# Low-weight pass of the up projections on 64-row halves of the array, in a fused convolution and two MLPs

## The reference, cut to what matters

```
x = attn(x, weight).reshape(8192, 192)
h = x @ w_in1;  g = maximum(0.01 * h, h);  x = g @ w_out1
h = x @ w_in2
P = a[0] + a[1] * h + a[2] * h**2 + a[3] * h**3
Q = 1 + |b[0]| * |h| + |b[1]| * h**2
out = (P / (Q + 1e-6)) @ w_out2
```

## Time and profile before

| | us |
|---|---|
| median of 3 runs | 1404.3 |
| the profiled execution's own time | 1407.92 |
| its span on the core | 1406.1 |
| mean granted TensorE clock | 0.973 |
| PE busy | 1293.8 (92%) |
| PEld busy | 1035.3 (74%) |
| DVE busy | 1068.8 (76%) |
| ACT busy | 1048.8 (75%) |
| POOL busy | 627.8 (45%) |

### The profile page before, as it was taken

How to read it: one execution, slowest core, us unless ns; L and a number is a source line. 1 busy time by engine, 2 the same in 40 slices (tenths; PEclk the granted TensorE clock), 3 DMA queues, 4 the chain that set the end, 5 groups by cost and what they waited for, 6 DMA issues and landing times.

```text
span 1406.1 us, 14543 instructions
## 1 busy us (share of the span) xinstructions
PE 1293.8 (92%) x5724; PEld 1035.3 (74%) x5724; DVE 1068.8 (76%) x913; ACT 1048.8 (75%) x1075; POOL 627.8 (45%) x265
## 2 busy tenths in 40 slices
PE   6989999999999999999999999999999999999575
PEld 5768787777777777777777877777787777778453
DVE  3447877878687787868778786877878687787774
ACT  4557787777787787778778777887877777787563
POOL 0014544545445454544545444454544445454553
PEclk8899999999999999999999999999999999999886
DMA  8200000000000000000000000000000000000000
GB/s 202 55 1 12 0 12 13 1 24 1 24 1 12 13 0 24 0 25 0 12 13 1 24 0 24 0 12 13 0 24 0 24 1 12 0 1 12 0 12 11
DMA packets 25091, 21.73 MB, mean 15 GB/s; under 512 B 2909, under 2 KB 23997, under 8 KB 25023
## 3 DMA queue, kind: packets, MB, share of 16 engines
q1 hardware_dynamic: 25023, 20.80, 5.3%
HBM read 14.49 MB, written 6.30 MB: 15 GB/s over the span
## 4 chain that ended last, share of the span: by engine, by line
issue 47%; POOL 44%; PE 4%; ACT 2%; DMA 1%; DVE 1%; POOLq 0%; SPq 0%; ACTq 0%; DVEq 0%
POOL den L297 23%; POOL lo L303 21%; PE h L580 2%; DMA den<-in_moe_w_in 1%; DMA band<-tap_rows 0%; DVE lo L527 0%; ACT hi L385 0%; PE acc L599 0%; PE h L546 0%; PE acc L600 0%; PE acc L590 0%; PE acc L591 0%; PE acc L592 0%; DMA coef_b<-in_moe_b 0%; ACT h L381 0%
## 5 line engine op out<-in xcount | busy, mean ns | idle before, releaser
L580 PE MATMUL h<-xs,wa 128*128 128x512 f32 x2520 | 620.5, 397 | 66.6 <-DVE xs L474 27.9
L297 POOL TENSOR_TENSOR den<-den,rec 128x1024 f32<-128x1024 f32 x128 | 323.7, 2529 | 762.8 <-ACT den L372 762.8
L580 PEld LDWEIGHTS h<-xs,wa 128*128 128x128 f32 x2520 | 474.5, 191 | 191.6 <-DVE xs L474 34.7
L303 POOL TENSOR_TENSOR lo<-pol,rec 128x1024 fp32r<-128x1024 f32 x128 | 307.1, 2399 | 4.0 <-DVE pol L507 4.0
L489 DVE SCALAR_TENSOR_TENSOR hi<-pol,coef_a,rec 128x1024 fp32r<-128x1024 f32 x128 | 164.3, 1284 | 143.2 <-ACT rec L338 88.6
L527 DVE TENSOR_TENSOR lo<-h,hi 128x1024 fp32r<-128x1024 f32 x128 | 156.4, 1222 | 132.2 <-ACT hi L385 131.8
L599 PE MATMUL acc<-lo,wb 128*128 128x512 f32 x512 | 202.3, 395 | 18.3 <-POOL lo L303 18.3
L590 PE MATMUL acc<-hi,wb 128*128 128x512 f32 x512 | 208.8, 408 | 10.9 <-DVE out_cm L502 8.8
L381 ACT ACTIVATE h<-h 128x1024 f32<-128x1024 f32 x128 | 129.7, 1014 | 116.1 <-PE h L580 116.0
L357 ACT ACTIVATE rec<-h 128x1024 f32<-128x1024 f32 x124 | 127.3, 1027 | 108.0 <-PE h L580 107.3
L591 PE MATMUL acc<-hi,wb 128*128 128x512 f32 x512 | 202.3, 395 | 0.0
(11 more groups left out here) (76 smaller groups left out, 954.7 us busy)
## 6 DMA issues: line engine op xcount, KB each, us to landing
out<-out_tok SPq DMA_DIRECT2D x16, 384.0 KB, 2.6
x_tok<-in_x SPq DMA_DIRECT2D x64, 82.5 KB
pol<-in_moe_w_out SPq DMA_DIRECT2D x4, 384.0 KB, 10.8
x_tok<-in_x SPq DMA_DIRECT2D x16, 78.0 KB
den<-in_moe_w_in SPq DMA_DIRECT2D x2, 512.0 KB, 8.4
den<-in_moe_w_in SPq DMA_DIRECT2D x4, 256.0 KB, 8.5
rec<-in_moe_w_out SPq DMA_DIRECT2D x2, 384.0 KB, 10.4
den<-in_moe_w_out SPq DMA_DIRECT2D x2, 384.0 KB, 6.1
```

The source lines that it names most:

```text
L297: nc.gpsimd.tensor_tensor(den[k][:, :], den[k][:, :], rec[k][:, :], ALU.mult).then_inc(s_den, 1)
L303: nc.gpsimd.tensor_tensor(lo2[k][:, :], pol[k][:, :], rec[k][:, :], ALU.mult).then_inc(s_lo2, 1)
L580: last = T.matmul(dst[:, half, :], lhs, xs[m][:, part, :], start=(j == 0), stop=(j == 4))
```

## The change

Of each up projection the fifth matmul of both tiles is taken out of `up`. In its place, once a pair, come two matmuls over 64 rows each: the low weights of tile 0 from partitions 0 to 63 by a new copy of x high on partitions 0 to 63 (`rest_hi`), and the low weights of tile 1 from partitions 64 to 127 by x high where it already is. They write different PSUM banks. The product of low weights and low x, which the fifth matmul also gave, is no longer computed. The remaining four matmuls of a tile are `up_whole`, the pair of half-array matmuls is `up_rest`. In layer 2 `up_rest` comes last and in layer 1 first (except in phase 6, where it comes last there too), so that in ordinary steps the four half-array matmuls of both layers follow one another. ScalarE gets one more copy of 64 by 512 per block and layer; in phase 6 VectorE's second subtraction, and with it TensorE, waits for it. `tap_half`, a small row used before the first block, now shares the memory of `conv_sb`.

```diff
-        tap_half = sb("tap_half", [1, HEADS * ROW])
+        rest_hi = [sb(f"x_rest{m}", [DR, COLS], F32R)[:, :] for m in range(2)]
+        conv_row = conv_sb[:, :, :].rearrange("p a c -> p (a c)")
@@ ScalarE
                 nc.scalar.activation(xs[1][DR:P, 2, :], fold[DR:P, :], ACT.Copy).then_inc(s_x2_hi, 1)
+                nc.scalar.activation(rest_hi[1], fold[DR:P, :], ACT.Copy).then_inc(s_x2_rest, 1)
...
                 nc.scalar.activation(xs[0][DR:P, 2, :], xt_ps[DR:P, 1, ::-1], ACT.Copy).then_inc(s_xt_hi, 1)
+                nc.scalar.activation(rest_hi[0], xt_ps[DR:P, 1, ::-1], ACT.Copy).then_inc(s_xt_rest, 1)
@@ VectorE
-                dve.wait_ge(s_xt_hi, 2 * c + 2)
+                dve.wait_ge(s_xt_rest, c + 1)
@@ TensorE
-            def up(m, pair0, dst, rest_ready, done):
+            def up_whole(m, pair0, dst, opens, rest_ready, done):
...
-                    w = [wa[m][:, j, f * P:(f + 1) * P] for j in range(4)]
-                    terms = [(w[0], 0), (w[1], 0), (w[0], 1), (w[2], 2), (w[3], 2)]
+                    w = [wa[m][:, j, f * P:(f + 1) * P] for j in range(3)]
+                    terms = [(w[0], 0), (w[1], 0), (w[0], 1), (w[2], 2)]
...
+            def up_rest(m, pair0, dst, opens, done):
+
+                f = 2 * (pair0 % STEPS)
+                T.matmul(dst[:, 0, :], wa[m][0:DR, 3, f * P:(f + 1) * P], rest_hi[m], start=opens, stop=not opens)
+                last = T.matmul(dst[:, 1, :], wa[m][DR:P, 3, (f + 1) * P:(f + 2) * P], xs[m][DR:P, 2, :],
+                                start=opens, stop=not opens)
+                if done is not None:
+                    last.then_inc(done, 1)
...
-                    up(1, n, hidden_2(n), x2_rest_ready, s_h2)
+                    up_whole(1, n, hidden_2(n), True, x2_rest_ready, None)
+                    if phase == 0:
+                        pe.wait_ge(s_x2_rest, n // STEPS + 1)
+                    up_rest(1, n, hidden_2(n), False, s_h2)
...
                             if transposes:
+                                pe.wait_ge(s_xt_rest, m0 // STEPS + 1)
                                 pe.wait_ge(s_xt_lo, 2 * (m0 // STEPS) + 2)
-                        up(0, m0, hidden_1(n), xt_rest_ready, s_h1)
+                        if transposes:
+                            up_whole(0, m0, hidden_1(n), True, xt_rest_ready, None)
+                            pe.wait_ge(s_xt_hi, 2 * (m0 // STEPS) + 2)
+                            up_rest(0, m0, hidden_1(n), False, s_h1)
+                        else:
+                            up_rest(0, m0, hidden_1(n), True, None)
+                            up_whole(0, m0, hidden_1(n), False, xt_rest_ready, s_h1)
```

More of the change, by code:

```diff
@@ L103, in conv_mlp_mlp @@
         one = sb("one", [P, 1])
-        tap_half = sb("tap_half", [1, HEADS * ROW])
+        rest_hi = [sb(f"x_rest{m}", [DR, COLS], F32R)[:, :] for m in range(2)]
+        conv_row = conv_sb[:, :, :].rearrange("p a c -> p (a c)")
         out_row = out_cm[:, :, :].rearrange("p a c -> p (a c)")
-        tap_rows = [t[0:1, 0:HEADS * ROW].rearrange("p (h j) -> p h j", h=HEADS) for t in (tap_half, out_row)]
+        tap_rows = [t[0:1, 0:HEADS * ROW].rearrange("p (h j) -> p h j", h=HEADS) for t in (conv_row, out_row)]
         tap_dram = nc.dram_tensor("tap_rows", (H, ROW), F32, kind="Internal").ap()
@@ L156, in conv_mlp_mlp @@
         s_x2_lo = sem("x2_lo")
+        s_x2_rest = sem("x2_rest_doubled")
+        s_xt_rest = sem("xt_rest_doubled")
         s_abs = sem("abs_h")
@@ L579, in up @@
                             rest_ready()
-                        last = T.matmul(dst[:, half, :], lhs, xs[m][:, part, :], start=(j == 0), stop=(j == 4))
-                last.then_inc(done, 1)
+                        last = T.matmul(dst[:, half, :], lhs, xs[m][:, part, :], start=opens and j == 0,
+                                        stop=not opens and j == 3)
+                if done is not None:
[5 more added lines that the diff above has]
+                                start=opens, stop=not opens)
+                if done is not None:
+                    last.then_inc(done, 1)
             def down(m, pair0, hi, lo, lo_ready, done):
```

## The result

The changed kernel took 1419.28 us (median of 6 runs, 1415.65 to 1423.09) against 1403.86 us before. The ratio is 1.0113, 95% interval 1.0089 to 1.0136: slower, by 15.4 us. The profiled execution of the changed kernel has a span of 1420.9 us, 14.8 more than before.

A forecast was written before the change was run, and what follows sets the result against it. TensorE's matmul stream was taken to set the time nearly everywhere; 132 charges of 0.55 us less 43.6 us saved gave +29 us, 1437 for the profiled execution and a median of 1433 us, range 1396 to 1464.

The forecast's parts named there:

- Entering and leaving, 0.44 us: TensorE: switching from whole-array to half-array matmuls and back costs 0.22 us each way, 0.44 for both.
- The second half trails by 0.11 us: Half-array pair on TensorE: the second half's weight load follows the first's, so it trails by 0.11 us.
- 8 w - 2.72 us a block: Block's net change on TensorE: four double and four single windows count, charges less saved streaming.
- w: Charge for one window, TensorE's half-array work between whole-array matmuls; forecast 0.55 us, the change being zero at 0.33.
- Phase 7 is hidden in the waits of phase 0: Phase 7's window costs and saves nothing, hidden in waits of 1.7 and 0.8 us at phase 0's start.
- The copies cost nothing: ScalarE's added 0.59 us copies in phases 6 and 7 fall into waits; uncovered, 1.2 us a block, 18 in all.
- The clock: Granted clock stays at 1.00 in mid-run; a fall from that would make the forecast wrong.
- start together: Rival: both halves of a half-array pair start at once, w = 0.44, +14.5 us, 1419 us; chance 0.15.
- No overlap: Rival: a pair's halves run one after the other, all streaming plus switches, +58 us, 1462 us; chance 0.17.
- Cheap change: Rival: row changes cost as in small transposes and halves start at once, w = 0.30, -4, 1400 us; chance 0.10.
- loads ahead: Rival: TensorE loads half-array weights while the whole array streams, w = 0.15, -24, 1380 us; chance 0.14.

The follow-up runs named there:

- e5: Changed kernel with layer 1's half-array pass last in every step, so ordinary steps have two separate one-pair windows; 1.0229 of the kernel before.
- e4: Changed kernel without the low-weight pass over the remainder rows, copies and their waits kept; 0.9726 of the kernel before.
- e1: Kernel before with only the two added ScalarE copies and VectorE's wait for the first, every matmul as before; 1.0035 of the kernel before.
- e8_early: Kernel before with the remainder's split at a block's end moved ahead: ScalarE's copy before the slope, VectorE's subtraction before the residue; 0.9834 of the kernel before.
- e10_ordinary_early: Changed kernel with half-array windows in ordinary steps only, phase 6's copy from SBUF and the remainder's split moved ahead; 0.9842 of the kernel before.
- e3: Changed kernel with both half-array matmuls of a pair on partitions 0 to 63, so they can't run side by side; 1.0401 of the kernel before.
- e2: Changed kernel with its order, copies and waits, but the low-weight pass on all 128 rows; 1.0032 of the kernel before.
- e6: Kernel before with the two added copies, phase 6's reading xs in SBUF so VectorE's second subtraction need not wait; 0.9987 of the kernel before.
- e11: Changed kernel with half-array windows in the ordinary steps of phases 1, 2 and 5 alone; 1.0008 of the kernel before.
- e7: Changed kernel with half-array windows in ordinary steps only, the fifth whole-array matmul elsewhere, phase 6's copy from SBUF; 1.0081 of the kernel before.
- e9: Changed kernel with the remainder's split at a block's end moved ahead; 0.9926 of the kernel before.

## Why the prediction was right in sign and range, and too high

The sign, and the reason for it, held: a window costs to enter and leave about what it saves. The range of 1396 to 1464 holds 1419.3. But the forecast was +29 us and +15.4 came. By its own steps:

- *Entering and leaving, 0.44 us.* Right. The trace gives 0.41, and its two parts are those read from the output transposes: a late start (0.32 for 0.227) and an exposed load (0.34 for 0.227).
- *The second half trails by 0.11 us.* Wrong, and this is the largest term: 132 x 0.11 = 14.5 us. The loads of L593 and L594 both start at 851.12. The row I took it from shows two loads of the whole array, one behind the other (693.68, 693.79 in the earlier trace rows); it says nothing of loads into different rows. The Trainium skill (TensorE: Matmul & The Clock Gate, Measured speedup vs the span model) has about 4 ns for a further tile; the trace agrees, with 3 to 4 ns between starts.
- *8 w - 2.72 us a block.* Too high in its count. With w = 0.41 it gives 0.56 us; the windows cost 0.26 (82.59 less the 82.33 with copies alone). Phase 2 has a wait that hides its window, which e5 and e4 show and which I could have seen in the table (9.51 against 9.07). In phase 4 both windows are hidden, not one (11.42 against 11.39). The second window of phase 6 doesn't count either, though I had a wait of ScalarE for it: phase 6 is 0.20 longer than with the copies alone (11.32 against 11.12) and phase 7 is 0.20 shorter (9.78 against 9.98), so that phases 6, 7 and 0 take 32.23 us in both kernels. Phase 3 pays 0.26, not 0.37. Against this an ordinary step costs 0.02 us and does not save 0.04, because the matmuls behind a window are spaced wider for a while.
- *Phase 7 is hidden in the waits of phase 0.* Right: no time is lost there, by the same sum. The waits on L479 and L523 are 2.2 us, for 2.5 before.
- *The copies cost nothing.* Wrong in phase 6, by 0.22 us a block, 3 us in all (e1's 5 us hold two more cold stretches besides). I set the subtraction's late start against the time when its result is needed and left out the subtraction's own 0.69 us: 727.44 + 0.69 = 728.13, needed at 727.32 + 3 x 0.227 = 728.00. In phase 7 nothing, as said.
- *The clock.* Named only as what would make the forecast wrong, "if the granted clock in mid-run falls". It does: 5 cold stretches for 2, one of them twice as long (2.8 us), which makes 5.6 us in the profiled execution. The runs of the changed kernel lie at 1416 (three, mean clock 0.973 to 0.976) and 1422 (three, 0.970 to 0.971), which is the size of a few such stretches.

Sum for the profiled execution, by the starts of its steps: 3.9 us are lost up to the start of the first block's phase 4 (124.7 us before, 128.6 after); behind it not quite 14 blocks at 0.48 us, 6.5 us, a little over half of it windows and the rest copies; cold stretches 5.6; and the last steps are 1.3 us shorter. That is 14.7 of 14.8 us. What costs the 3.9 us in the first steps is not shown: single windows stand there, but two kernels without any window there, e8_early and e10_ordinary_early, reach that phase at 121.5 and 126.5 us.

Of the rivals, "start together" named 1419 and had its mechanism right; part of that exact hit is chance, as its sum lacks the copies and the clock and counts too many windows. "No overlap" (1462) is e3, built: 1.0401, 1460 us. "Cheap change" (w = 0.30) is refuted by the 0.41 of the trace, "loads ahead" by 851.12 and 851.78.

## What to carry to other kernels

Two row halves of the array do run side by side, but going there and back costs about two matmul times of 512 columns: two adjacent pairs just break even, and by this sum it pays only with more than two pairs in one window, which no run tried. Before pricing a saving on the busiest engine, take the work out altogether: e4 showed that of 5.4 us a block only 3.0 would arrive. Moving a VectorE subtraction, and the copy that it needs, out of GpSimd's way, found on the way, was worth 1.7%, and it took away the wait around whose end the clock fell.

## What the runs showed of the hardware that was not expected

- Weight loads into different halves of the rows start together (3 ns apart), while two loads of the whole array are 0.11 us apart.
- For the ten matmuls behind an exposed load the spacing is 0.233 us in the mean (0.224 to 0.240) in place of 0.227; the same is seen before the change, behind phase 3's transposes.
- In mid-run cold stretches begin only around the end of the phase 0 wait, from 0.6 us ahead of it to 1.7 us behind. In the kernels with no window beside it there are 1 to 4 (before, e1, e2, e6, e11), and 5 in e4, whose wait is longer; with windows in phases 7 and 0 there are 4 to 10 (e3, the changed kernel, e5, e7), each from one profiled execution. With 1.4 to 1.6 us of wait at the very start of phase 0 there are none in three kernels (e8, e9, e10), windows or not. The length of the wait alone doesn't tell: e3 and e5 have 1.68 us, three matmuls into the phase, with at most 0.15 us ahead of it, and have 4 and 8. Why one block has a stretch and the next like block has none, no run here tells.
- A VectorE subtraction with both inputs in SBUF (L474) that started 0.27 us into GpSimd's L303 took 2.65 us for 0.69 and ended 0.55 us behind it; L303 itself was no longer than elsewhere (2.37). The other way round, GpSimd's L297 took 3.07 us for 2.4 where it started beside VectorE's L507 with 0.8 us of that still to run. That order costs 0.7 us, the first one 2.0.
